# Four small reorderings in the attention stage of a one-core attention and MLP kernel

## The reference

```python
keep = is_global | is_local             # 8 global keys, 96 local ones
scores = where(keep, scale * q @ k.T + bias, -1e9)
a = exp(scores - max); a = a / (sum(a) + 1e-9)
x = a @ v                               # attention, x: [2, 768, 512]
u = x + ((x.T @ U) @ V).T               # tokens mixed through rank 32
y = u + relu(u @ w_ch1) @ w_ch2         # 2048 hidden
h = relu(y @ w_in)                      # then a gated layer with a 768 x 768
out = (u2 * (w_spatial @ norm(v2) + b)) @ w_out
```

## Time and profile before

| | before |
|---|---|
| median of 3 runs | 507.07 us (507.07 to 509.49) |
| the profiled execution | 506.97 us |
| its span in the profile | 505.0 us |
| PE busy | 496.5 us, 98% |
| DVE, ACT, POOL busy | 285.8, 213.8, 208.8 us |

### The profile page before, as it was taken

How to read it: one execution, slowest core, us unless ns; L and a number is a source line. 1 busy time by engine, 2 the same in 40 slices (tenths; PEclk the granted TensorE clock), 3 DMA queues, 4 the chain that set the end, 5 groups by cost and what they waited for, 6 DMA issues and landing times.

```text
span 505.0 us, 7871 instructions
## 1 busy us (share of the span) xinstructions
PE 496.5 (98%) x2822; PEld 413.9 (82%) x2822; DVE 285.8 (57%) x666; ACT 213.8 (42%) x490; POOL 208.8 (41%) x178
## 2 busy tenths in 40 slices
PE   8999999999999999999999999999999999999997
PEld 7787577787888888888888888888888998889995
DVE  5887688521259376564655565648687356531530
ACT  7978678542235443342342322414654113331121
POOL 6896656354335676744565636423430000000000
PEclk9999999999999999999999999999999999999999
DMA  8810800122222421022222021031500000110002
GB/s 241 282 62 18 298 23 1 45 84 84 83 84 86 165 83 55 30 83 84 83 85 83 1 83 47 27 104 32 177 1 1 1 0 22 43 62 1 1 22 104
DMA packets 14552, 36.28 MB, mean 72 GB/s; under 512 B 2480, under 2 KB 2480, under 8 KB 14512
## 3 DMA queue, kind: packets, MB, share of 16 engines
q1 hardware_dynamic: 12640, 32.35, 18.9%
q10 hardware_dynamic: 1872, 3.41, 1.8%
HBM read 32.61 MB, written 3.15 MB: 71 GB/s over the span
## 4 chain that ended last, share of the span: by engine, by line
PE 93%; ACT 2%; DVE 2%; issue 1%; DMA 1%; SPq 0%; ACTq 0%; DVEq 0%
PE bank L1212 23%; PE bank L1487 15%; PE bank L1419 9%; PE bank L1341 9%; PE bank L1516 9%; PE bank L1509 9%; PE bank L1549 6%; PE bank L1265 4%; PE bank L1247 3%; PE bank L1232 3%; PE bank L1283 1%; ACT prob L944 1%; PE bank L1288 1%; DMA qk_raw<-in_qk 1%; DVE prob L597 1%
## 5 line engine op out<-in xcount | busy, mean ns | idle before, releaser
L462 POOL TENSOR_TENSOR w_slot<-stage,w_slot 128x1024 fp32r<-128x1024 f32 x30 | 73.0, 2444 | 65.6 <-ACT w_slot L1010 65.6
L776 DVE TENSOR_TENSOR uT<-bank,uT 128x512 f32<-128x512 f32 x68 | 45.8, 689 | 25.3 <-PE bank L1516 23.3
L944 ACT ACTIVATE prob<-prob,row_min 128x256 f32<-128x256 f32 (+1 forms) x96 | 46.0, 480 | 13.6 <-DVE row_min L597 13.5
L1212 PE MATMUL bank<-sp_slot,vn 128*128 128x384 f32 x288 | 50.3, 334 | 0.0
L1212 PEld LDWEIGHTS bank<-sp_slot,vn 128*128 128x128 f32 x288 | 50.0, 188 | 0.2
L1487 PE MATMUL bank<-u_op,s_slot 128*128 128x512 f32 x192 | 47.6, 389 | 0.0
L1419 PE MATMUL bank<-hid,w_slot 128*128 128x512 f32 x192 | 47.0, 393 | 0.0
L1341 PE MATMUL bank<-u_split,w_slot 128*128 128x512 f32 x192 | 46.4, 391 | 0.0
L1516 PE MATMUL bank<-hid,w_slot 128*128 128x512 f32 x192 | 46.1, 389 | 0.0
L1509 PE MATMUL bank<-hid,w_slot 128*128 128x512 f32 x192 | 46.1, 389 | 0.0
L1419 PEld LDWEIGHTS bank<-hid,w_slot 128*128 128x128 f32 x192 | 35.7, 188 | 8.2 <-issue 0.9
(11 more groups left out here) (121 smaller groups left out, 832.5 us busy)
## 6 DMA issues: line engine op xcount, KB each, us to landing
stage<-in_w_ch SPq DMA_DIRECT2D x32, 512.0 KB, 3.3
qk_raw<-in_qk SPq DMA_DIRECT2D x23, 256.0 KB, 4.6
v_all<-in_v SPq DMA_DIRECT2D x12, 256.0 KB, 4.9
out_dram<-o_stage ACTq DMA_DIRECT2D x12, 256.0 KB, 2.0
stage<-in_w_spT SPq DMA_DIRECT2D x6, 384.0 KB, 2.9
stage<-in_w_in SPq DMA_DIRECT2D x4, 512.0 KB, 3.9
stage<-in_w_out SPq DMA_DIRECT2D x2, 512.0 KB, 3.5
V_raw<-in_V SPq DMA_DIRECT2D x4, 96.0 KB, 4.4
```

The lines of the kernel that those rows point to most:

```text
L462: nc.gpsimd.tensor_tensor(dst[:, LO, :], stage[n % 2][:, 0:w], dst[:, HI, :].bitcast(F32), ALU.subtract).then_inc(w_lo, 1)
L776: vec.tensor_tensor(y, y_bank(e)[:], y, ALU.add).then_inc(y_sum, 1)
L944: last = sc.activation(prob[r][:, e, 0:w], prob[r][:, e, 0:w], ACT.Exp, bias=row_min[:, k:k + 1], scale=-1.0, accum_out=row_sum[:, q:q + 1])
L1212: last = mm(out_ap, lhs(a), rhs(c), start=(n == 0), stop=(n == 3 * len(terms) - 1))
```

## The change

Six edits, all in the attention stage. No instruction is added or taken away.

1. DVE: `take_oT(12)` and `take_oT(13)` move from the start of steps 13 and 14 to between the halves of `score_bias` of steps 12 and 13 (the list `OT_AMID`; quads 0 and 1 were there already).
2. ACT: `take_xT` of steps 12 and 14 moves ahead of `exps(s+2, 0)`.
3. ACT: `round_z(0)` moves ahead of `take_probT(14)`.
4. The fourth `mix` (step 21) writes score bank 0 and not `aux`. So `turn_o` waits for three `sum_u` at most, and the fourth `sum_u` moves on DVE from the end of step 21 to the end of step 22.
5. PE: in step 22 `turn_x(10)` moves behind `weigh(22)`.
6. POOL: the second half of `split_early(0)` moves from step 13 to step 16.

```diff
         def mix_bank(j):
 
+            if j == FIRST - 1:
+
+                return s_bank[0]
             return o_bank if j >= 2 * KD and j % 2 else aux
+
+
+
+        OT_AMID = (0, 1, 12, 13)
...
-                    if g in (10, 13):
-                        split_early(0, g // 13)
+                    if g in (10, 16):
+                        split_early(0, g // 16)
...
-                    if s >= 3:
+                    if s >= 1 and s - 1 not in OT_AMID:
                         take_oT(s - 1)
...
-                    if s in (0, 1):
-
+                    if s in OT_AMID:
                         score_bias(s + 2, 0)
                         take_oT(s)
                         score_bias(s + 2, 1)
...
-                    if s in (15, 17, 19, 21):
+                    if s in (15, 17, 19):
                         sum_u((s - 15) // 2)
+                    if s == 22:
+                        sum_u(FIRST - 1)
...
+                    if s == 14:
+
+                        round_z(0)
                     if s >= 2:
                         take_probT(s)
                     if s == 13:
                         copy_z(0)
-                    if s == 14:
-                        round_z(0)
...
+                    if s in (12, 14):
+
+                        take_xT((s - 2) // 2)
                     if 0 <= s + 2 < QUADS:
                         exps(s + 2, 0)
-                    if s >= 2 and s % 2 == 0:
+                    if s >= 2 and s % 2 == 0 and s not in (12, 14):
                         take_xT((s - 2) // 2)
...
-                    pe.wait_ge(u_sum, min(s - 14, 8) // 2)
+                    pe.wait_ge(u_sum, min(s - 14, 6) // 2)
...
-                    if s >= 2 and s % 2 == 0:
+                    if s >= 2 and s % 2 == 0 and s < QUADS - 2:
                         t = (s - 2) // 2
                         pe.wait_ge(x_half, 2 * t + 2)
                         turn_x(t)
...
                     if s >= 0:
                         weigh(s)
+                    if s == QUADS - 2:
+                        pe.wait_ge(x_half, s)
+                        turn_x(TILES - 2)
```

## The result

| | before | changed |
|---|---|---|
| median | 507.07 us (506.99 to 509.49) | 504.57 us (504.45 to 505.53) |
| runs | 7 | 7 |
| profiled execution | 506.97 us | 504.57 us |
| span | 505.0 us | 502.6 us |
| PE busy | 496.5 us | 495.5 us |

The ratio is 0.9946, with a 95% interval of 0.9931 to 0.9962: 2.5 us less. The forecast was 504.7 us, with a span of 502.65 us.

The account below looks back on a forecast made before the run. TensorE bounds the kernel (93% of the chain): its work plus its gaps. Gains of 1.78 + 0.57 = 2.35 us take profiled 506.97 to 504.62, median 504.7 us; range 504.0 to 506.0.

Parts of the forecast that it names:

- Gaps, not work: Whole kernel: edits are worth only the TensorE gaps they close; what is saved ahead of 98 us is kept behind.
- restarts: TensorE pieces after a wait run slightly longer (turn_o 0.41 to 0.44 us, not 0.37); some 0.5 us at most overall.
- Step 12: Before turn_o(12): ScalarE's take_xT(5), not VectorE's oT, comes last; moving it ahead gains 0.82 us, 0.86 with the restart.
- Step 13: Before turn_o(13): VectorE's oT copy between the halves of the minima gains 0.29 us, 0.36 with the restart.
- Step 14: 0.41 us gained before turn_o(14); round_z(0) first, worth 0.3 to 0.4 us beside other edits, starts weigh(14) at 61.93, 0.01 us spare.
- The middle: Steps 12 to 14 together gain 1.78 us with restarts, carried unchanged through steps 15 to 21.
- The end: Steps 22 and 23: waits before turn_x(10) (0.59) and weigh(23) (0.22) go, 0.2 us before weigh(22)'s second half comes; 0.57 us gained.
- The POOL move: GpSimd, step 16: the moved 1.28 us split fits 1.30 us of idle and costs nothing; weight load at about 69 us.
- On which side of 0.5%: Whole time against a bound of 504.53 us, 2.5 us from no change: faster 0.36, same 0.59, slower 0.05.
- the lower bound: Whole time if all gaps and some 0.5 us of restarts go: at most 2.85 us gained, so 504.2 us.

Follow-up runs that it names:

- the one with the early copy: Changed kernel with ScalarE's last copy of turned probabilities that weigh(22) waits for moved between the halves of the last exponentials; median 504.94 us.

## Why the prediction was right

The mechanism held, and so did the sum: 2.35 us forecast, 2.40 in the spans, 2.5 in the medians. Part of how closely it held is luck: in step 14 and at the end, errors of 0.1 to 0.2 us cancel. By its own steps:

- Gaps, not work. The first product of the MLP stage came 2.40 us earlier (97.95 to 95.55) and the span ended 2.4 us earlier, so what was saved before 98 us was kept behind it. TensorE's busy time also reads 1.0 us less (496.5 to 495.5), but 0.5 of that is the filler at the very start of the program (4.64 us before, 4.17 in this trace), which no edit touches; the changed kernel's second profile has 496.0 us busy in the same span. So some 0.5 us is busy time, about what the prediction allows for restarts, and 1.9 us is waiting.
- Step 12: ScalarE's `take_xT(5)` as the true releaser of `turn_o(12)`. Shown by the kernel without edit 2: the gap is back at 0.82 us with VectorE's copy early. The two xT copies cost 1.4 us when put back, where the gaps alone are 0.82 + 0.41 = 1.23; the restarts, 0.1 us in the timelines, are part of the difference.
- Step 13: 0.29 us and some restart. The kernel without edit 1 costs 0.5, as expected of it, and 0.2 of that stands before `turn_o(12)`.
- Step 14: `round_z` first was given 0.3 to 0.4 us, only beside the others; it measured 0.4. Mis-sized was the margin: `weigh(14)` was to start without a gap, with 0.01 us to spare, and TensorE stands still for about 0.1 us there (61.83, the end of turn_x, to 61.95). ScalarE's exponentials run to 60.69, with the last piece overlapping `round_z`, which starts at 60.59 when ScalarE is free and not, as laid out, when the fold has ended. The total does not show it, since the pieces ahead had come 1.31 us earlier (turn_x, 62.49 to 61.18 in the timelines) and not 1.22; `weigh(14)` started 0.02 us from its forecast of 61.93.
- The middle: 1.78 forecast, 1.83 found at the scores of step 15 (66.12 to 64.29) and again at the turn of step 22 (91.65 to 89.82), so steps 15 to 21 carry the gain unchanged. From 66 to 89 us TensorE is busy for 22.93 of 23.00 us, as from 68 to 91 before.
- The end: 0.57 forecast, 6.30 less 5.73 found, 0.57. Of its terms, the 0.59 us before turn_x went and the 0.20 us before the second half of `weigh(22)` came, as laid out. Two others did not. The first half of `weigh(22)` was to find its copy no later than the end of `turn_o(21)`, and waits 0.22 us for it; and of the 0.22 us before `weigh(23)` 0.03 were to be left, and 0.17 are. Both times the layout has 0.05 us from the end of VectorE's copy to TensorE's start, and 0.14 to 0.15 were measured (91.20 to 91.35, 94.38 to 94.52). What made up for it: `turn_o(21)` came 0.93 us behind its turn and not 1.11 as before, where the layout has 0.03 us of gain and the list of terms 0.1; and `turn_o(22)` started at 93.94, which is 95.77 in the old clock, 0.23 us ahead of the 96.0 laid out. The size of the end is right by errors that cancel.
- The POOL move: zero, and measured zero. In step 16 the moved split takes 1.28 us, as before in step 13, and VectorE's instructions beside it (0.41, 0.68, 0.42 us) are as long as in the kernel before. By the Trainium skill (SBUF — State Buffer, "Who interferes with whom") a VectorE instruction with two SBUF inputs contends with a GpSimd instruction that reads SBUF. The trace agrees as far as it goes: VectorE's instructions there read at most one operand from SBUF, and neither kind took longer. No run here tests a pair that should interfere. The weight load behind the split went out at 68.74 us, about 69 in the forecast, and TensorE waits for no weights from 98 to 188 us.
- On which side of 0.5% it would fall the prediction had put 0.59 on no change. The measured gain is 0.54%, with an interval from 0.38 to 0.69, so the bound lies inside it and neither side is shown.
- Two sums of the prediction are off by 0.02 us, and nothing rests on them: 56.11 + 1.43 + 0.91 is 58.45 and not 58.47, and the gaps and restarts of the lower bound add up to 2.83 us and not 2.85.

## What to carry to other kernels

Where one engine is busy 98% of the time, list its gaps one by one, and for each gap compute the end of every instruction that the waiting one needs: the name in the wait list can be the wrong one, and here it was for the largest gap. Then walk the new order by hand as far as the next engine's queue, since a closed gap can make the next one: by the rows of before `round_z` had no gap to close, and it was worth 0.4 us beside the other edits. The prices of edits to one stall are not added up: taken back one by one the two at the end cost 0.10 and 0.33 us, together 0.58. And a total that comes out right does not show that its terms were; compare each with its row.

## What the runs showed of the hardware

The longer executions start with TensorE at about half its pace for longer. The profiles of two kernels, at the first scores and at the ten matmuls of filler behind them, first of the changed kernel (504.57 us):

```profile
6.33 1.56 PE L1244 MATMUL bank<-qk_split 64*128 64x128 f32 x24 [0.62 <-DVE qk_split L587]
7.82 1.38 PE L1216 MATMUL bank<-ident 128*128 128x128 f32 x10
```

then of the kernel without edit 5, in an execution of 507.59 us:

```profile
6.39 2.82 PE L1244 MATMUL bank<-qk_split 64*128 64x128 f32 x24 [0.21 <-DVE qk_split L587]
9.14 2.50 PE L1216 MATMUL bank<-ident 128*128 128x128 f32 x10
```

The same instructions take 1.8 times as long, until about 14 us, and every later row is shifted by some 2.6 us. The granted clock reads 1.00 in both stretches, so this loss of pace does not show there; it looks like the lower of TensorE's two levels (1.2 and 2.4 GHz), which is an inference from the durations. All profiles start TensorE alike, with twenty matmuls of filler from 1.54 us on. In the three longer ones these take 4.63 to 4.64 us; in the ten others they take 4.04 to 4.64, and in one of them the scores behind still take 2.04 us and not 1.56, so that there the pace rises somewhere between the end of the filler and 8 us. TensorE's idle time between filler and scores does not tell the two kinds apart: 0.21 us or nothing listed in the longer ones, from nothing listed to 0.70 us in the others. What decides, no run here tells. Ten of the 100 executions of the changed kernel and its variants but one were of this kind, and 5 of 12 of the one with the early copy, whose edit changes nothing that runs before 88 us; an experiment on a tenth of a microsecond has to compare like with like.

Five executions are of a third sort, one each of the kernel before, the changed kernel, the one without edit 1, the one without edit 3 and the one with the early copy: 1.0 to 1.2 us above the rest, with a mean granted clock of 0.996 or 0.997 over the span, where every other execution on record has 0.999 or 1.000. The highest time in the result's table, 505.53 us, is one of them. None was profiled, so where in the program the clock was lower is open.
